# The split of attention weights, a fetch and the join of two stages in a three-stage set-attention kernel

## The reference

```python
# attention: x (2, 12480, 128), inducing (32, 128)
h = mab(I, x)             # 32 queries over 12480 tokens, softmax, times x
y = mab(x, h)             # 12480 tokens over 32 rows of h: softmax(x h^T / sqrt(C)) @ h

# first MLP, rational activation, 24960 tokens, d_ff 2048
h = y @ w_in
g = (a0 + a1*h + a2*h**2 + a3*h**3) / (1 + |b0|*|h| + |b1|*h**2 + 1e-6)
z = g @ w_out

# second MLP
h = z @ w2_in
out = (h * cos(h)) @ w2_out
```

## Time and profile before

| | us |
|---|---|
| median of 3 runs (2580.45 to 2585.31) | 2583.31 |
| the profiled execution, its own time | 2584.47 |
| its span, first to last instruction | 2582.70 |
| first stage and join | about 0 to 110 |
| second stage | about 110 to 1430 |
| third stage | about 1430 to 2582 |
| busy: PE, DVE, ACT, POOL | 2549.2, 2332.2, 2446.8, 2162.4 |

### The profile page before, as it was taken

One profiled execution on the slowest core, in us unless ns is written; L12 is line 12 of the kernel. 1 busy time (PEld: TensorE's weight loads), 2 busy tenths in 40 slices (PEclk: granted clock), 3 DMA queues, 4 the chain that ended last, 5 costly groups with the idle time before them and its releaser, 6 DMA issues.

```text
span 2582.7 us, 38783 instructions
## 1 busy us (share of the span) xinstructions
PE 2549.2 (99%) x10790; PEld 1806.7 (70%) x10790; DVE 2332.2 (90%) x2712; ACT 2446.8 (95%) x3152; POOL 2162.4 (84%) x1471
## 2 busy tenths in 40 slices
PE   7899999999999999999999999999999999999999
PEld 5566666566666656565656688888888888888887
DVE  4899999999999999999999888888888888888887
ACT  5699999999999999999999999999999999999998
POOL 0499999999999999999999888888888888888886
PEclk9899999999999999999999999999999999999999
DMA  7200000000011000000000000000000000000000
GB/s 212 73 8 11 8 11 8 11 8 11 8 35 54 12 8 11 8 12 8 11 8 5 17 12 12 12 11 11 11 11 11 11 11 11 11 11 11 11 11 15
DMA packets 27815, 48.92 MB, mean 19 GB/s; under 512 B 3352, under 2 KB 12344, under 8 KB 27512
## 3 DMA queue, kind: packets, MB, share of 16 engines
q1 hardware_dynamic: 27768, 48.33, 6.4%
HBM read 18.04 MB, written 12.78 MB: 12 GB/s over the span
## 4 chain that ended last, share of the span: by engine, by line
PE 62%; POOL 14%; issue 10%; DVE 8%; ACT 4%; DMA 1%; POOLq 1%; SPq 0%; DVEq 0%; ACTq 0%
PE bank L1251 22%; PE bank L1243 21%; POOL work L423 9%; PE bank L1082 8%; PE bank L1089 8%; DVE work L816 5%; POOL work L412 3%; POOL part_hi L433 2%; ACT work L575 2%; DVE bank L795 1%; PE bank L1234 1%; ACT work L564 1%; POOL part_hi L427 1%; PE bank L1010 1%; DVE work L804 1%
## 5 line engine op out<-in xcount | busy, mean ns | idle before, releaser
L490 POOL TENSOR_TENSOR act_lo<-work,act_hi 128x960 fp32r<-128x960 f32 (+1 forms) x413 | 832.2, 2015 | 195.5 <-ACT act_hi L658 195.4
L1089 PE MATMUL bank<-work,v 128*128 128x480 f32 x1664 | 740.9, 567 | 0.2 <-ACT tokens_t L582 0.2
L1082 PE MATMUL bank<-part_hi,stack_now 96*128 96x480 f32 x2496 | 664.7, 399 | 8.4 <-DVE work L816 2.4
L423 POOL TENSOR_TENSOR work<-work 128x960 f32<-128x960 f32 x278 | 622.4, 2239 | 40.3 <-POOL work L412 3.0
L974 DVE SCALAR_TENSOR_TENSOR work<-work,bank 128x960 f32<-128x960 int32 x416 | 479.3, 1152 | 141.6 <-ACT work L645 141.5
L1082 PEld LDWEIGHTS bank<-part_hi,stack_now 96*128 96x128 f32 x2496 | 433.6, 189 | 238.2 <-DVE work L816 165.0
L795 DVE SCALAR_TENSOR_TENSOR bank<-bank,over_c,work 128x960 f32<-128x960 f32 x416 | 508.4, 1222 | 41.8 <-PE bank L1082 33.4
L816 DVE SCALAR_TENSOR_TENSOR work<-bank,coef_a,work 128x960 f32<-128x960 f32 x416 | 502.3, 1208 | 0.2 <-PE bank L1082 0.2
L559 ACT ACTIVATE work<-work,made 128x960 f32<-128x960 f32 x416 | 469.0, 1128 | 26.9 <-POOL work L423 26.9
L980 DVE TENSOR_TENSOR work<-work,bank 128x960 f32<-128x960 f32 x416 | 477.4, 1148 | 0.0
L1089 PEld LDWEIGHTS bank<-work,v 128*128 128x128 f32 x1664 | 309.9, 189 | 211.0 <-issue 187.5
(11 more groups left out here) (120 smaller groups left out, 2950.2 us busy)
## 6 DMA issues: line engine op xcount, KB each, us to landing
x_group<-tokens_t SPq DMA_DIRECT2D x52, 240.0 KB, 2.2
out_dram<-work SPq DMA_DIRECT2D x52, 240.0 KB, 2.4
x_ring<-in_x_dram SPq DMA_DIRECT2D x28, 240.0 KB, 5.3
work<-in_x_dram SPq DMA_DIRECT2D x24, 240.0 KB, 4.1
w_raw<-in_moe_w_in_dram SPq DMA_DIRECT2D x2, 1024.0 KB, 10.2
stack_now<-first_hi SPq DMA_DIRECT2D x8, 192.0 KB, 3.8
stack_now<-next_hi SPq DMA_DIRECT2D x16, 96.0 KB, 2.2
stack_now<-first_lo SPq DMA_DIRECT2D x4, 192.0 KB, 5.4
```

Of the source, the lines that this page charges most:

```text
L423: nc.gpsimd.tensor_tensor(quot[k % 3], square[k % 3], abs_h[k % 3], ALU.add).then_inc(den_ready, 1)
L490: nc.gpsimd.tensor_tensor(act2_lo[:, k % 2, w], angle[k % ANGLES][:, w], act2_hi[:, k % 2, w].bitcast(F32), ALU.subtract).then_inc(act2_pa ...
L1082: mm = pe.matmul(place_out[:, t, :], stack_now[:, i, w], part_hi[0:K3, place, :], start=start, stop=stop, skip_group_check=not start)
L1089: mm = pe.matmul(sums, v[:, 2 * u + t, :], g[:, t * GROUP:(t + 1) * GROUP], start=(2 * u + t == 0), stop=(2 * u + t == CHUNKS - 1))
```

## The change

1. The parts of the attention weights are made before they are turned. `norm_s2` normalises in place (120 x 128 in `att_exp`) one unit earlier, `invert` goes from place 3 to place 1 of the same unit, and POOL's new `part_att` writes high, high, low into `att` (120 x 4 x 2 x 32 and 120 x 4 x 32). PE turns the finished parts; `keep_att` writes them from `spare` straight into `part_hi`. `high_att`, `low_att` and `att_t` are gone.
2. `fetch_group(0)` is issued by SP ahead of the x loads that wait for `h_summed`, not behind them.
3. At the join PE's first `hidden`, `turn_att(1)`, `total(1)` change places; DVE and ACT likewise.
4. Scratch tiles lie at other addresses.

```diff
-SUM, INVERT, NORM, TURN = (-12, 3), (-11, 3), (-10, 3), -9
-KEEP_ATT, HIGH_ATT, LOW_ATT = (-8, 3), -7, -6
+SUM, INVERT, NORM, PART_ATT = (-12, 3), (-11, 1), (-11, 3), -10
+TURN, KEEP_ATT = -9, (-8, 3)
...
             sp.dma_start(w_raw, w_in).then_inc(w1_loaded, 16)
-            for q in range(RING, GROUPS - STEP_GROUPS):
-                load_group(q)
...
+            sp.wait_ge(xt_ready, 1)
+            fetch_group(0)
+            for q in range(RING, GROUPS):
+                load_group(q)
...
-            def high_att(place):
-
-                nc.gpsimd.tensor_copy(part_hi[0:K3, place, :], att_t[0:K3, :]).then_inc(att_hi_ready, 1)
-
-            def low_att(g, place):
-
+            def part_att(g):
+
+                high = att_exp[:, :, 0:M].rearrange("p j (o m) -> p j o m", o=1).broadcast_to([SUB, GROUP_SUBS, 2, M])
+                nc.gpsimd.tensor_copy(att[:, :, 0:2, :].bitcast(F32R), high).then_inc(att_hi_ready, 1)
                 pool.wait_ge(att_hi_ready, g + 1)
-                low = part_hi[2 * M:K3, place, :]
-                nc.gpsimd.tensor_tensor(low, att_t[2 * M:K3, :], low.bitcast(F32), ALU.subtract).then_inc(att_parted, 1)
-                pool.wait_ge(att_parted, g + 1)
+                nc.gpsimd.tensor_tensor(att[:, :, 2, :].bitcast(F32R), att_exp[:, :, 0:M], att[:, :, 0, :], ALU.subtract).then_inc(att_parted, 1)
...
-            pool.wait_ge(att_kept, 1)
-            high_att(0)
-            low_att(0, 0)
+            pool.wait_ge(att_ready, 1)
+            part_att(0)
+            pool.wait_ge(att_ready, 2)
+            part_att(1)
...
-                nc.vector.tensor_tensor(att[:, :, :, :], thrice, inv, ALU.mult).then_inc(att_ready, 1)
+                nc.vector.tensor_tensor(att_exp[:, :, 0:M], att_exp[:, :, 0:M], inv, ALU.mult).then_inc(att_ready, 1)
...
-                nc.vector.tensor_copy(att_t[0:K3, :], spare[0:K3, 0:GROUP]).then_inc(att_kept, 1)
+                nc.vector.tensor_copy(part_hi[0:K3, place, :], spare[0:K3, 0:GROUP]).then_inc(att_kept, 1)
```

66 lines of the change are left out of this document (27 added, 39 removed).

## The result

| | before | changed |
|---|---|---|
| median of the runs | 2583.73 us (4 runs, 2580.45 to 2585.31) | 2558.97 us (4 runs, 2556.54 to 2559.59) |
| profiled execution, its span | 2584.47, 2582.7 us | 2556.54, 2554.7 us |
| mean granted clock | 0.996 | 0.999 |

The ratio is 0.9904, with a 95% interval of 0.9887 to 0.9921: 24.8 us faster, where 21 to 22 were forecast. A second set of runs gave 2558.30 us and 0.9911 (0.9894 to 0.9927).

A forecast was written before the change was run, and what follows sets the result against it. Bound by a ring: quotient, slope's two matmuls, product, next quotient, 3.14 us per undisturbed unit. Loop -16.0, w2 steps +3.2, fetch -4.2, join -4.2 make -21.2 from 2584.47; 2562 us forecast (2556 to 2568), range 2550 to 2574.

The forecast's parts named there:

- POOL's stall: Loop: ACT stands idle for POOL's denominator, late behind `low_att`; one quotient distance is 0.26 us too long: -0.26 per group.
- normalisation: Loop, DVE: from 384 elements to 120 x 128, about 0.27 us shorter, short enough to fit behind the absolute: -0.14 per group.
- reciprocal: Loop, DVE: moved between product and quotient, its whole price delays the next quotient; 0.07 to 0.17, taken as +0.09 per group.
- steps on w2: Last 12 groups: one DVE step behind k = 7 waits for POOL's denominator; 3.6 us less 0.4 at k = 1: +3.2.
- fetch: First stage: PE's `x_group` wait goes (-4.06), clock -1.0, later x +0.9 (27.4 instead of 26.5): -4.2 us (0 to -5.5).
- join: Join: sums run while PE would stand, `spread_peak` 4.9 earlier, first quotient at 98.3 instead of 102.57: -4.2 us (0 to -7).
- The free room: Loop, DVE: 0.31 us free behind the absolute before the product can start; none between product and quotient.
- The pair of POOL: Loop: POOL's new cast and subtraction take about 0.8 us (0.5 to above 1.8); lateness of 0.56 worked off within three units.
- Rival (a): Loop: POOL's cast and subtraction take 1.2 to 1.4 us, holding ACT 0.1 to 0.2 per group: 2573 us; chance 0.08.
- Rival (e): Loop: POOL's cost goes by runs of 32; gain used up at 1.7 us, 2590 at 2.5 us; chance 0.04.
- The rule against the change: Loop: two-SBUF-input DVE steps and POOL's SBUF reads exclude each other; normalisation could cost a good part of a denominator per group.
- rival (b): Loop: normalisation meets a denominator in every group, waits 0.4, product 0.3 late: 15 us on top, 2577; chance 0.05.

The follow-up runs named there:

- the dose run: Changed kernel with POOL's low-part subtraction made three times in a row, against the changed kernel: 2605.26 us, 26.53 us per group.

## Why the prediction was right, step by step

| step | predicted | measured |
|---|---|---|
| POOL's stall, per group | -0.26 | -0.265 |
| normalisation | -0.14 | -0.145 |
| reciprocal | +0.09 | +0.087 |
| other units | 0 | -0.08 |
| steps on w2, in all | +3.2 | +3.9 |
| the loop, in all | -12.8 | -15.6 |
| layout, ahead of the loop | 0 | -3.8 in the profile, alone |
| fetch | -4.2 | -3.3 (-1.3 to -5.9), alone |
| join | -4.2 | -2.2 (-3.9 to +0.8), alone |
| counted twice | 0 | +3.3 in the profile |
| sum | -21.2 | -24.8, the whole in the medians |

The rows of the first part come from different executions and don't add up to the last line.

**The loop.** The unit in which both the stall ended and the reciprocal now stands went from 3.405 to 3.226 us in the mean; 3.139 is what it is without the reciprocal (the run with it moved), which splits the two. The unit that the normalisation left went from 3.283 to 3.138. What failed is the term of the loop as a size: it took every unit that the change doesn't touch to stay as it was. Three fell by a little: `keep_att`'s from 3.409 to 3.383, the next from 3.165 to 3.132, and the one behind the reciprocal from 3.139 to 3.118. Together 0.08 us, 4 us in 49 groups. The last of them is 3.140 again in the run with the norm later, where no reciprocal stands ahead of it: the reciprocal's price is given back in part, like that of the two w2 steps. What the first two were held by wasn't tried.

**The free room.** The prediction read 0.31 us free behind the absolute, and none between product and quotient. The runs bear it out: behind the absolute 0.17 alone is free, 0.28 alone is free and 0.45 costs 0.09, and between product and quotient 0.17 costs 0.09.

**The pair of POOL.** The size was estimated at 0.8 by element count and is 0.86. The step behind it was weaker than it looked: that POOL's lateness of 0.56 would not reach ACT is true by 0.12 us only. Rival (a), a pair of 1.2 to 1.4 us, was put at 0.1 to 0.2 us per group; by the dose run it would have been 0.2 to 0.4. Rival (e) was to use up the change's gain at 1.7 us, with 0.7 paid of each us; by the dose the loop's gain is gone at 1.4, with all of it paid. It didn't happen, as the pair is short; but it was nearer than said. Its 2590 for a pair of 2.5 us was also mis-added: 1.4 us beyond 1.1, at 0.7, over 50 groups are 49 us on top of 2562, so 2611. The dose run measured 2605.26 at 1.90 us already.

**The rule against the change.** The norm takes 0.28 us in all 49 groups, so rival (b) did not happen, for the reason given: it starts just behind a denominator's end. The Trainium skill, SBUF — State Buffer, § Who interferes with whom, has the rule by which it would; the trace of the run with the norm one step earlier agrees with that rule, with 0.65 us for 0.28, in a time that is 26.5 us longer. The margin was put at the 0.1 of the reciprocal; it is 0.06.

**The w2 steps.** Behind k = 7 they take 0.75 and 0.83 us, and cost 0.36 us per group where 0.3 was written; the meeting at k = 1 is gone (0.28).

**The fetch.** The wait of 4.06 us went. Forecast was -4.06 + 0.9 = -3.2 at `score2(0)` and -1.0 of clock behind it. Measured is -4.3 at `score2(0)` in the mean, of which 3.5 at equal clock and the rest by executions that had no drop at 28 us, a thing the sum did not know. Behind it the low clock from 63.95 to 67.37 is gone (1.00 in the fetch run), and the first `hidden` comes 1.4 us sooner (22.81 us behind `score2(0)` instead of 24.21), near the 1.0. The +0.9 us for a later x was not seen (26.75 against 26.77 us in the mean), and the sign that was named, x at 27.4, failed: it is 26.23 in the changed kernel's profile.

**The join.** The 4.2 us are there in the run of the order alone, as 3.9 at the first quotient, for the reason given (`peak_all` ahead of the first denominator). That the layout alone would take the same 2 us away was not seen: it too changes what POOL's first denominator waits for. So the first part of the program brought 12.0 us in the profiled executions (8.4 forecast), of which some 3 are luck, since in the medians it is 24.8 - 15.6 = 9.2. That 9.2 is near 8.4 is in part luck as well: the layout's 3.8 us had no term, and 3.3 us were counted twice.

## What to carry to other kernels

A step on a busy engine has no price of its own: find the ring that sets the pace, then the room in each of its units. In this loop one step of up to 0.28 us behind each absolute was free. Where a neighbour's work is shortened to end a stall, measure what is left to spare behind it with a dose, since a pair of 0.86 us was free here and one of 1.9 cost more than the change had brought. And where two edits remove the same wait, their prices don't add; run each alone and in pairs, and read the start-up from several executions.

## What was not expected of the hardware

Which of VectorE's steps stand while POOL works goes by their form in these traces. In the changed kernel the reciprocal of 120x4 starts while POOL works in all its 50 places of the loop and takes 0.168 us, and the absolute, from the bank, takes 0.64 to 0.66 us in all 414 cases in which it starts inside a denominator. In the kernel before, `shift_s2` (L757), as large as the norm and the same operation but with one input from the bank, starts beside POOL 50 times and takes 0.28 us. But the norm, `part_sum` and `chosen` stand (0.65, 1.93 and 1.10 us for 0.28, 0.16 and 0.30), and so does the copy of a single row.

The wait for x at 26 us goes with 3.3 us in the start of `score2(0)`: in the five executions in which PE stood idle there for 0.89 to 1.31 us, the granted clock stayed at its 2.4 GHz level; in the six with 2.19 to 3.63 us of idle time it was at the 1.2 GHz level for 3.4 us, in one of them 6.8, beginning between 0.8 us ahead of the wait's end and 1.7 us behind it. Half of the 3.3 us is x itself, which comes 1.7 us later in these six (27.51 against 25.84 us), and half the lower clock. With the early fetch both cases occur; the three profiles without it show only the second.
